# Experts' loops turned round: from 512 tokens by all of w1 to 1,024 tokens by half of w1

## The reference

```python
    logits = x @ w_gate
    logits = logits - logits.max()
    P = np.exp(logits)
    for _ in range(8):
        P /= P.sum(1, keepdims=True) + 1e-09
        P /= P.sum(0, keepdims=True) + 1e-09
        P *= N / E
    out = np.zeros((N, D), dtype=np.float32)
    for e in range(E):
        h = np.maximum(x @ w1[e], 0.0)
        ye = h @ w2[e]
        out += P[:, e:e + 1] * ye
```

## Time and profile before

| | |
|---|---|
| median of 3 runs | 2385.5 us |
| the profiled execution's own time | 2386.86 us |
| its span | 2385.1 us |
| TensorE matmuls busy | 2261.7 us, 95% |
| VectorE busy | 1559.6 us, 65% |
| ScalarE busy | 981.6 us, 41% |
| GpSimd busy | 461.0 us, 19% |
| mean DMA rate | 56 GB/s |

### The profile page before, as it was taken

The page is one execution under the profiler, slowest core; times in us unless marked ns, Lnnn a source line. Parts: engine busy times, 40 slices in busy tenths (PEclk is TensorE's granted clock), DMA queues, the critical chain, the costliest instruction groups (busy, mean ns, idle before and its releaser), DMA issues.

```text
span 2385.1 us, 43991 instructions
## 1 busy us (share of the span) xinstructions
PE 2261.7 (95%) x16891; PEld 2241.0 (94%) x16891; DVE 1559.6 (65%) x2953; ACT 981.6 (41%) x1675; POOL 461.0 (19%) x325
## 2 busy tenths in 40 slices
PE   2689999999999989999999999999999999999999
PEld 2689999999999889999999999999999999999999
DVE  6898888888874685555556666555556655565553
ACT  2455555555555433333333433333333333333331
POOL 0000000000000312222222222122222222222221
PEclk9799999999999999999999999999999999999999
DMA  3211111111112310011112211110013211111101
GB/s 105 84 33 48 49 49 49 49 50 49 50 37 71 120 54 24 31 54 54 55 54 93 94 54 54 55 53 25 32 54 117 70 54 54 54 54 54 54 1 27
DMA packets 73194, 132.46 MB, mean 56 GB/s; under 512 B 5608, under 2 KB 36584, under 8 KB 72936
## 3 DMA queue, kind: packets, MB, share of 16 engines
q1 hardware_dynamic: 72936, 129.14, 16.4%
HBM read 114.96 MB, written 14.16 MB: 54 GB/s over the span
## 4 chain that ended last, share of the span: by engine, by line
PE 81%; DVE 10%; ACT 7%; issue 2%; DMA 0%; DVEq 0%; ACTq 0%; SPq 0%
PE bank L1431 13%; PE bank L1433 13%; PE bank L1432 13%; PE bank L1598 11%; PE bank L1599 11%; PE bank L1600 11%; PE bank L1412 2%; PE bank L1418 2%; PE bank L1417 2%; PE bank L1422 1%; ACT ubuf L648 1%; ACT ubuf L650 1%; PE bank L1407 1%; ACT ubuf L646 1%; DVE tmp L861 1%
## 5 line engine op out<-in xcount | busy, mean ns | idle before, releaser
L1431 PE MATMUL bank<-x_h,w_h 128*128 128x256 f32 x2112 | 595.8, 282 | 9.0 <-issue 4.1
L1433 PE MATMUL bank<-x_h,w_l 128*128 128x256 f32 x2112 | 595.0, 282 | 0.0
L1432 PE MATMUL bank<-x_l,w_h 128*128 128x256 f32 x2112 | 594.1, 281 | 0.0
L1598 PE MATMUL bank<-w_h,h_h 128*128 128x384 f32 x1536 | 518.2, 337 | 0.4 <-DVE acc L1233 0.4
L1600 PE MATMUL bank<-w_h,h_l 128*128 128x384 f32 x1536 | 515.0, 335 | 0.0
L1599 PE MATMUL bank<-w_l,h_h 128*128 128x384 f32 x1536 | 514.9, 335 | 0.0
L567 POOL TENSOR_TENSOR h_l<-u_s,h_h 128x512 fp32r<-128x512 f32 x192 | 244.6, 1295 | 1136.6 <-ACT h_h L778 1136.6
L1431 PEld LDWEIGHTS bank<-x_h,w_h 128*128 128x128 f32 x2112 | 400.7, 190 | 11.9 <-issue 6.0
L1432 PEld LDWEIGHTS bank<-x_l,w_h 128*128 128x128 f32 x2112 | 401.9, 190 | 0.0
L1433 PEld LDWEIGHTS bank<-x_h,w_l 128*128 128x128 f32 x2112 | 401.5, 190 | 0.0
L1240 DVE SCALAR_TENSOR_TENSOR acc<-bank,prob,acc 128x384 f32<-128x384 f32 x168 | 103.5, 616 | 370.6 <-PE bank L1600 370.6
(11 more groups left out here) (164 smaller groups left out, 4035.8 us busy)
## 6 DMA issues: line engine op xcount, KB each, us to landing
stage<-w_ SPq DMA_DIRECT2D x48, 768.0 KB, 7.9
w_raw<-w_ SPq DMA_DIRECT2D x96, 384.0 KB, 4.8
qb<-q_in_ SPq DMA_DIRECT2D x24, 192.0 KB
kb<-k_in_ SPq DMA_DIRECT2D x24, 192.0 KB
vb<-v_in_ SPq DMA_DIRECT2D x24, 192.0 KB
x_hi<-x2h_s SPq DMA_DIRECT2D x36, 128.0 KB, 1.8
x_lo<-x2l_s SPq DMA_DIRECT2D x36, 128.0 KB, 1.8
x_h<-x_hi SPq DMA_DIRECT2D x6, 768.0 KB, 4.4
```

What stands on the lines that cost most here:

```text
L1431: pe.matmul(dst, w[0], x[0], start=first, stop=False)
L1432: pe.matmul(dst, w[0], x[1], start=False, stop=False)
L1433: return pe.matmul(dst, w[1], x[0], start=False, stop=last)
L1598: pe.matmul(dst, h_h[:, f, t_], w2s[slot][0][:, f], start=n == 0, stop=False)
```

## The change

- `HT` is 512 and covers 1,024 tokens in the two column blocks of a product. A group j is now all 1,024 tokens of a pass by one half (`QUADS` = 2, 512 columns) of an expert's w1. A product's two quarters stay, but each covers 128 columns, and each term is one matmul of 512 columns for each of the three part pairs.
- w1 has one buffer for each half j (`w1s`). The sums and low parts for group g+1 are made in the y block of group g: `w1_sums` ahead of the add of k = 0, `w1_lo` in three parts, ahead of the adds of k = 2, 3 and 4.
- w2 is held once. Its half for group g+1 is loaded when the y block of group g-1 is done. `w2_hi` and `w2_lo` follow `w1_hi` in every group.
- A y block has eight blocks k of 128 tokens, with four column blocks f each, in `F_ORDER` (1, 0, 3, 2): 12 matmuls of 384 columns per k. There are 16 adds for each expert instead of eight.
- x2 has a second buffer, used by the next pass. `xt_sums` of the next pass stands ahead of the add of k = 0 in the first group of the pass's last expert, `xt_lo` ahead of the add of k = 4 in the second.
- At the hand-over the x2 sums are of 1,024 tokens and stand at m = 4, `xt_lo` at m = 6, and only the first half of w1 is made. The steps of the normalisation are spread over more of the first two groups, and `sink_columns` has one instruction less.

```diff
-M_ORDER = (2, 3, 0, 1)
+M_ORDER = (4, 5, 6, 7, 0, 1, 2, 3)
+F_ORDER = (1, 0, 3, 2)
...
-            def product(name, j, terms):
+            def product(name, j, ps, terms):
                 q = int(name[3])
-                for i in range(2):
-                    to = h_bank[name][:, i * HT:(i + 1) * HT]
-                    for n, (w, x) in enumerate(terms):
-                        mm = three(to, (w1h[:, q, w, i], w1l[:, q, w, i]), (x2s[j][0][:, x], x2s[j][1][:, x]),
-                                   n == 0, n == len(terms) - 1)
+                for n, (w, x) in enumerate(terms):
+                    mm = three(h_bank[name][:], (w1s[j][0][:, w, q], w1s[j][1][:, w, q]),
+                               (x2s[ps % 2][0][:, x], x2s[ps % 2][1][:, x]), n == 0, n == len(terms) - 1)
                 mm.then_inc(h2_step, 1)
...
-            def y_block(ex, j, slot):
-                g = ex * GP + j
+            def y_block(ex, j):
+                g = ex * QUADS + j
...
+                pe.wait_ge(w2_low, (g + 1) * NW2)
                 for k, m in enumerate(M_ORDER):
...
+                    if zero and k in (3, 5, 7):
+                        sum_of_columns(k // 2 - 1)
+                    if one and k in (2, 4, 6):
+                        sum_of_columns(4 + k // 2)
+                    if k >= 2 or not zero:
+                        pe.wait_ge(acc_done, g * PB + k - 1)
...
+                    for n, f in enumerate(F_ORDER):
+                        if k == 0:
+                            pe.wait_ge(hl_done, g * len(LOW) + n + 1)
+                        if k == 4 and n % 2 == 0:
+                            pe.wait_ge(hl_dve, g * len(LOW_DVE) + n + 2)
...
# VectorE, group
+                for k in range(PB):
+                    if k == 0 and (nxt or j == 0):
+                        w1_sums(ex + j, g + 1, 1 - j)
+                    if x2_next and k == 4 * j:
+                        (xt_sums, xt_lo)[j](x2_next)
+                    if first and k in (4, 6):
+                        sink_columns(k // 2 - 2)
+                        sink_rows(k // 2 - 1)
+                    if second and k in (3, 5, 7):
+                        sink_columns(5 + k // 2 - 1)
+                        if k < 7:
+                            sink_rows(6 + k // 2 - 1)
+                    if (nxt or j == 0) and 1 < k < 5:
+                        w1_lo(g + 1, 1 - j, (k - 2,))
                     add_expert(g, j, k, ps, e)
...
# load queue
+            def load_w1(ex, e, j):
+                if not isinstance(ex, int) or ex:
+                    sp.wait_ge(w1_low, ((ex - 1) * QUADS + j) * 3 + 3)
+                sp.dma_start(stages[j][:], w1_dram[e, :, :, j * QF:(j + 1) * QF]).then_inc(w1_in[j], 16)
+
+            def load_w2(ex, e, j):
+                if not isinstance(ex, int) or ex:
+                    sp.wait_ge(y2_full, ((ex - 1) * QUADS + j + 1) * PB)
...
+                    load_expert(e0 + E, 0)
+                    store_out(ps)
+                    load_expert(e0 + E + 1, 1)
+                    if ps + 2 < PASSES:
+                        load_x2(ps + 2)
...
# VectorE at the hand-over
                 if m == 1:
-                    w1_sums(0, 0)
-                    xt_sums(0, 0)
+                    w1_sums(0, 0, 0)
                 if m == 2:
                     w1_lo(0, 0)
                 if m == 4:
-                    xt_lo(0, 0)
-                    w1_sums(0, 1)
+                    xt_sums(0)
                 if m == 6:
-                    w1_lo(0, 1)
+                    xt_lo(0)
```

More of the change, by code:

```diff
@@ L1313, in group @@
                 if second:
-                    sink_rows(6)
-                if build:
-                    w1_sums(ex + 1, 0)
-                for k in range(B):
-                    if first:
-                        sink_columns(k)
-                        if k < 3:
-                            sink_rows(k + 1)
-                    if second and k < 2:
-                        sink_columns(6 + k)
-                        if k == 0:
-                            sink_rows(7)
-                    if build and k < 2:
-                        w1_lo(ex + 1, k)
-                    if build and k == 0:
-                        w1_sums(ex + 1, 1)
-                    add_expert(g, j, k, ps, e)
-                    if x2_next and k == 2:
-                        xt_sums(*x2_next)
@@ L1333, in group @@
-                if x2_next:
-                    xt_lo(*x2_next)
-            def expert(ex, ps, e, last=False):
-                for j in range(GP):
-                    zero = isinstance(ex, int) and ex == 0
-                    x2_next = (0, 1) if zero and j == 0 else (ps + 1, j) if last and ps + 1 < PASSES else False
-                    group(ex, j, ps, e, not last or ps + 1 < PASSES, x2_next)
+                    sink_rows(5)
+                for k in range(PB):
[12 more added lines that the diff above has]
+                        w1_lo(g + 1, 1 - j, (k - 2,))
+                    add_expert(g, j, k, ps, e)
@@ L1342, in _, with expert @@
+            def expert(ex, ps, e, nxt=True, x2_next=False):
+                for j in range(QUADS):
+                    group(ex, j, ps, e, nxt, x2_next)
             for ps in range(PASSES):
                 e0 = E * ps
+                more = ps + 1 < PASSES
                 expert(e0, ps, None)
                 if ps == 0:
-                    for i in range(GP * B):
-                        j, m = i // B, M_ORDER[i % B]
-                        dve.wait_ge(acc_done, i + 1)
-                        dve.tensor_scalar(acc[:, j * B + m], acc[:, j * B + m], prob[:, j * B + m, 0:1], None, ALU.mult)\
-                           .then_inc(scaled, 1)
@@ L1354, in _ @@
                     expert(e0 + 2 + 2 * r, ps, 2 + 2 * r)
-                expert(e0 + 7, ps, 7, True)
+                expert(e0 + 7, ps, 7, more, more and ps + 1)
         @block.tensor
@@ L1601, in y_block, with expert @@
                     mm.then_inc(y2_full, 1)
-            def expert(ex, slot, ps, first=False):
-                for j in range(GP):
-                    h_block(ex, j, ps, first)
-                    y_block(ex, j, slot)
+            def expert(ex, ps, first=False):
+                for j in range(QUADS):
+                    h_block(ex, j, ps, first and j == 0)
+                    y_block(ex, j)
             for ps in range(PASSES):
                 e0 = E * ps
-                expert(e0, 0, ps, True)
+                expert(e0, ps, True)
```

428 lines of the change are left out of this document (190 added, 238 removed).

## The result

The changed kernel takes 2412.7 us (median of 4 runs, 2411.26 to 2414.11) against 2385.8 us (2385.38 to 2386.51) for the kernel before, run beside it: a ratio of 1.0112, 95% interval 1.0095 to 1.013. It is slower by 26.9 us; the prediction said 19.5, and 2405 us. The profiled execution has a span of 2411.2 us, 26.1 more than before.

The account below looks back on a forecast made before the run. TensorE's matmuls, busy for 95% of the span, were taken as the bound. The terms -21.5 + 26.5 - 3.5 + 17 + 3 - 2 gave +19.5 us, so 2405 us against the median of 2385.5, range 2374 to 2420.

Parts of the forecast that it names:

- (a): Matmuls of 512 columns in the h blocks, 3,168 in place of 6,336 of 256: 21.5 us saved.
- The line's 0.2288: Straight line from 256 through 384 columns, giving 0.2288 us for a 512-column matmul against 0.2356 for a pair of 256.
- rival of cheap columns: Per-matmul overhead mostly goes at 512 columns: 0.2158 us each, 62.7 us saved, 2364 us in all; chance 0.13.
- The 15.8 us block of the earlier trace: 132 h matmuls taking 15.8 us with DMA queues at 200 GB/s, 0.28 more than otherwise; kept as unchanged.
- (c): Twice the adds on VectorE: 192 more of 0.61 us, 117 us in all, hidden beside TensorE.
- (d): Start of each y block: tenth matmul waits for GpSimd's second low part, 0.58 us a group, 26.5 us in 46 groups.
- (e): x2 sums at a pass end delay the add of k = 0: 6.4 us wait plus 2.0 slow clock, twice, 17 us.
- (f): `xt_lo` and `w1_lo`'s last part ahead of the add of k = 4 in the next group: 1.4 us, twice, 3 us.
- (g): The hand-over, with changed waits at m = 1 and m = 4 and in the normalisation: sum -2 us, from -8 to +8.
- Late stores: Next pass's first add waits for eight stores queued behind weights, 4 us late, twice: +12, 2417 us; chance 0.13.
- No GpSimd wait: Only the 0.25 us wait at k = 2 is left in each y block: +4.5, 2390 us; chance 0.14.

Follow-up runs that it names:

- Experiment 4: The changed kernel with each matmul of 512 columns made again as two of 256 into halves of the same bank: 2426.8 us.
- experiment 2: The changed kernel, but GpSimd makes the low parts of w2 only after VectorE has made those of w1: 2401.0 us, ratio 1.0062.
- experiment 1: The changed kernel, but in block k = 0 of each y block the eight high-part matmuls come before the four low-part ones: 2394.9 us, ratio 1.0037.
- the sweep: Not the kernel's computation: stretches of 24 fp32r matmuls on TensorE alone, an operand's address moved by 32 bytes each time; 117.1 to 123.3 ns at 256 columns.
- experiment 12: The kernel before with 320 bytes of padding ahead of w1, 64 ahead of `h_h` and 128 ahead of `x2_1`: 2371.9 us, ratio 0.9939.

## Why the prediction was right in sign and short in size

- **(a) Columns: -21.5 predicted (-20.6 for the 46 blocks measured), -23.3 measured, by luck in part.** The line's 0.2288 lies inside the 0.2267 to 0.2333 found. But the step "from 256 to 384 columns the distance grows by 0.0555" took 0.1178 for the price of 256 columns, and that price is 0.1133 where the arrays lie well. Experiment 4 has the changed kernel's addresses and matmuls of 256: by it 13.6 of the 23.3 us go with the width and 9.8 with the new addresses. The 13.6 are a mixture too: in passes 0 and 2 two halves cost 0.2398 against 0.2268 in one group of a pair, and 0.2266 against 0.2333 in the other. With both widths at their best, 2 x 0.1133 = 0.2266 and 0.2267, the width itself gives nothing. The rival of cheap columns (0.2158) is refuted; no placement came under 0.2267. The formula that the prediction quotes from the Trainium skill ("TensorE: Matmul & The Clock Gate", section "Back-to-back issue gap") is given there for an isolated matmul; for a stream with its weight loads the section says about 131 ns at 512 columns. The 226.7 to 233.3 ns measured agree with neither.
- **The 15.8 us block of the earlier trace rows** I put down to DMA traffic. That was wrong: placed, the same loads (some 213 GB/s) leave 14.96, and in the changed kernel an h block of pass 1 takes 15.11 us with 106 and with 310 GB/s beside it. It was the other buffer of x2.
- **(c) The adds are hidden, as said.**
- **(d) Right in place and chain, the total by luck in part.** 0.62 and 0.50 us lost at GpSimd's wait against 0.58; `w1_sums` and the add of k = 0 at the predicted times. All y blocks lose 52.0 - 30.2 = 21.8 us apart from the pass ends; 26.5 - 3.5 = 23 was said. But two things that were not foreseen make up for each other. The 41 ordinary y blocks now lie 0.69 us above 16.64 and not 0.58; in the j = 0 groups 0.24 of it are adds late behind the blocked `w1_lo`. And the six idle stretches of the kernel before, 5.1 us, are gone; without them its ordinary y blocks lost 3.7 us, where the prediction had 3.5.
- **(e), (f) Right in place, 20 us for 30.2.** The failed step is "each is some 0.61 and the block 6.7 us": it took 0.61 from VectorE's own rows and did not ask what GpSimd does beside it. The eleven sums took 10.0 us, 1290.69 to 1300.7. In (f) the wait is 2.24 and 1.78 us long and not 1.4, by the same blocking of the `w1_lo` ahead of `xt_lo`. Of the 10.2 us missing some 8 are these longer waits and 2.2 the clock: 14 and 17 matmuls at the lower level behind the first waits (14 was said), and 11 and 0 behind the second, where none was. Without the overlap (experiment 2) the eleven sums take 6.7 us, TensorE is 6.3 us late, and the four y blocks lose 20.5 us against their like: the forecast holds there.
- **(g)** -3.0 for -2 (its three terms add up to -2.5). The experts' stage begins 2.6 us later, where 1.5 was said, and the first two groups take 5.6 less, where 4 was said; about 1 us of this is their part of (a).
- **Late stores**: refuted, the first y blocks of passes 1 and 2 take 17.23 and 17.25 us. **No GpSimd wait**: refuted by the gap at the tenth matmul and by experiment 1's gain.

In sum: 23.3 + 3.0 gained, 52.5 lost. The 6.6 us between forecast and account are 10.2 too little at pass ends, less small errors of the other sign in (a), (d) and (g). The sign and most of the size come from the mechanisms that were named; that (a) and the total of (d) come so close is luck in part.

## What to carry to other kernels

Before giving VectorE or GpSimd more work, lay their timelines side by side: a VectorE and a GpSimd subtraction with all inputs in SBUF, 0.95 and 1.85 us when apart, took 2.58 us side by side, nearly the sum, and the one that an add waits behind is the one that hurts. Work for the next stage belongs in pieces behind the adds, not whole ahead of one: cutting it up gave 28.7 us here. Where the steady distance of matmul starts differs between twin blocks, a few bytes of padding are worth a try before loops are rebuilt, though no rule for choosing them came out of these runs: here 512 bytes of padding gave 33.2 us, and the rebuild with its orders mended 20.4.

## What the runs showed of the hardware that was not expected

- The distance of fp32r matmul starts at the full clock depends on where the arrays lie in SBUF: 0.1133 to 0.1199 us for 256 columns, 0.2267 to 0.2333 for 512, period 256 bytes in the sweep. 384 columns moved by 3 ns in the sweep; in the kernels they kept to 0.1733 in nearly all blocks, except in experiment 12, with 0.1746 and 0.1767 too.
- The rate can change at a late matmul inside one block, 0.1178 to 0.1133. Moving arrays that the block's matmuls don't read (`h_h` and those behind it) changed it. With the addresses fixed it went with the rate of the block before (22 of 22 blocks in experiment 12). The same placement gave 2352.6 us on two chips.
- VectorE's and GpSimd's mutual blocking: 0.95 to 2.58 us and a mean of 1.85 to 2.28 us for the same instructions.
